# Eight one-column VectorE instructions moved to later tiles, and three lists of waits put in another order, in a two-layer kernel on one core

## The reference

```python
# x: (2, 4096, 192) -> causal 7-tap convolution, one softmaxed set of taps for each of 8 groups of 24 channels
w = softmax(weight)                                  # (8, 7)
out[b, s, c] = sum_k w[c // 24, k] * x_padded[b, s + k, c]
x = out.reshape(8192, 192)
# layer 1
h = x @ w_in                                         # 192 -> 2048
g = h * clip(h + 3, 0, 6) / 6
x = g @ w_out                                        # 2048 -> 192
# layer 2
h = x @ w_in2
P = a[0] + a[1] * h + a[2] * h**2 + a[3] * h**3
Q = 1 + |b[0]| * |h| + |b[1]| * h**2
g = P / (Q + 1e-6)
return g @ w_out2
```

## Time and profile before

| | before |
|---|---|
| median of 3 runs | 1202.07 us |
| profiled execution, its own time | 1204.0 us |
| its span | 1201.9 us |
| PE busy in the span | 1186.5 us, 99% |
| VectorE (DVE) busy | 1160.7 us, 97% |
| ScalarE (ACT) busy | 1065.5 us, 89% |
| GpSimd (POOL) busy | 1072.9 us, 89% |
| granted TensorE clock, mean | 0.998 |

### The profile page before, as it was taken

One profiled execution on the slowest core, in us unless ns is written; L12 is line 12 of the kernel. 1 busy time (PEld: TensorE's weight loads), 2 busy tenths in 40 slices (PEclk: granted clock), 3 DMA queues, 4 the chain that ended last, 5 costly groups with the idle time before them and its releaser, 6 DMA issues. The chain is left out here.

```text
span 1201.9 us, 17842 instructions
## 1 busy us (share of the span) xinstructions
PE 1186.5 (99%) x5145; PEld 963.2 (80%) x5145; DVE 1160.7 (97%) x1784; ACT 1065.5 (89%) x1980; POOL 1072.9 (89%) x829
## 2 busy tenths in 40 slices
PE   8999999999999999999999999999999999999998
PEld 6778888888888888888888888888888888888754
DVE  7999999999999999999999999999999999998898
ACT  7888899898998988989998899889999899888886
POOL 5989989898998989999898998999989899898874
PEclk9999999999999999999999999999999999999999
DMA  4400000000000000010000000000000000000010
GB/s 147 152 2 10 1 23 1 23 10 23 1 1 24 9 23 1 1 32 1 22 1 15 17 2 23 1 23 10 1 23 1 23 1 1 14 1 14 1 44 13
DMA packets 11313, 22.02 MB, mean 18 GB/s; under 512 B 1744, under 2 KB 3152, under 8 KB 11216
## 3 DMA queue, kind: packets, MB, share of 16 engines
q1 hardware_dynamic: 10928, 20.89, 5.9%
q10 hardware_dynamic: 288, 0.01, 0.0%
HBM read 14.60 MB, written 6.29 MB: 17 GB/s over the span
## 5 line engine op out<-in xcount | busy, mean ns | idle before, releaser
L525 POOL TENSOR_TENSOR den<-den,sqr 128x512 f32<-128x512 f32 x246 | 360.7, 1466 | 92.3 <-ACT den L499 91.1
L599 POOL TENSOR_TENSOR g_lo<-g,g_hi 128x512 fp32r<-128x512 f32 x246 | 319.4, 1298 | 7.9 <-ACT g_hi L605 7.9
L492 POOL TENSOR_TENSOR g_lo<-r,g_hi 128x512 fp32r<-128x512 f32 x235 | 309.9, 1319 | 1.7 <-ACT g_hi L605 1.3
L605 ACT ACTIVATE g_hi<-g 128x512 fp32r<-128x512 f32 x246 | 155.9, 634 | 54.9 <-PE y1b_acc L385 47.1
L529 ACT ACTIVATE rsq<-den 128x512 f32<-128x512 f32 x246 | 155.0, 630 | 45.6 <-POOL den L525 42.7
L519 DVE SCALAR_TENSOR_TENSOR num<-h,monic,num 128x512 f32<-128x512 f32 x246 | 184.6, 751 | 8.2
L513 DVE SCALAR_TENSOR_TENSOR num<-h,monic,sqr 128x512 f32<-128x512 f32 x246 | 183.2, 745 | 0.0
L552 DVE SCALAR_TENSOR_TENSOR h<-num,monic,h 128x512 f32<-128x512 f32 x238 | 178.3, 749 | 0.2
L478 DVE SCALAR_TENSOR_TENSOR r<-r,h 128x512 f32<-128x512 f32 x235 | 160.4, 683 | 14.2 <-ACT r L471 13.4
L545 DVE SCALAR_TENSOR_TENSOR den<-den,h 128x512 f32<-128x512 f32 x238 | 161.9, 680 | 1.0 <-ACT h L541 0.9
L574 DVE SCALAR_TENSOR_TENSOR g<-den,h 128x512 f32<-128x512 f32 x238 | 161.1, 677 | 0.2
(11 more groups left out here) (182 smaller groups left out, 2886.8 us busy)
## 6 DMA issues: line engine op xcount, KB each, us to landing
stage_w<-w_pack SPq DMA_DIRECT2D x16, 448.0 KB, 3.4
raw_a<-x_a SPq DMA_DIRECT2D x16, 259.0 KB, 3.2
out<-y_a SPq DMA_DIRECT2D x16, 256.0 KB, 2.0
out<-y_b SPq DMA_DIRECT2D x16, 128.0 KB, 2.3
raw_b<-x_b SPq DMA_DIRECT2D x14, 129.5 KB, 2.7
r<-w_pack SPq DMA_DIRECT2D x4, 96.0 KB, 2.0
raw_b<-x_b SPq DMA_DIRECT2D x4, 65.5 KB, 4.6
y_a<-w_pack SPq DMA_DIRECT2D x2, 96.0 KB, 2.3
```

The source lines that it names most:

```text
L492: eng.tensor_tensor(g1_lo[t % 2][:, :], gated(t)[:, :], f32(g1_hi[t % 2][:, :]), ALU.subtract).then_inc(S["g1lo"], 1)
L525: eng.tensor_tensor(den_of(t), den_of(t), sqr_of(t), ALU.add).then_inc(S["den_sum"], 1)
L599: eng.tensor_tensor(g2_lo[t % 2][:, :], g2[t % 2][:, :], f32(g2_hi[t % 2][:, :]), ALU.subtract).then_inc(S["g2lo"], 1)
L605: return eng.activation(dst, src, ACT.Copy)
```

## The change

The seven entries of the set-up functions leave VectorE's START list, where they stood at the front (side, safe, inverse, c2), behind `gate1` (ratio, c01, scale) and belonged to steps 5, 6, 7, 8, 9, 10 and 11. They are now at the end of VectorE's BEGIN list, in steps 12 to 18. Three functions name their waits in another order.

```diff
-    "vector": [("monic_side", 5), ("monic_safe", 6), ("monic_inverse", 7), ("monic_c2", 8), ("gate1", 0), ("monic_ratio", 9),
-             ("monic_c01", 10), ("monic_scale", 11), ("conv_b1", AHEAD, (2, 2, 2, 3, 5, 6, 7), 1), ("g1lo", 1),
+    "vector": [("gate1", 0), ("conv_b1", AHEAD, (2, 2, 2, 3, 5, 6, 7), 1), ("g1lo", 1),
              ("conv_a", AHEAD, (0, 3, 5, 7, 8, 10))],
...
-             ("x2b_res", SUM1, 0), ("g1lo", 1), ("x2b_lo", SUM1, 0), ("conv_a", AHEAD, (6, 4, 4, 16, 4, 5))],
+             ("x2b_res", SUM1, 0), ("g1lo", 1), ("x2b_lo", SUM1, 0), ("conv_a", AHEAD, (6, 4, 4, 16, 4, 5)),
+             ("monic_side", 12), ("monic_safe", 13), ("monic_inverse", 14), ("monic_c2", 15), ("monic_ratio", 16),
+             ("monic_c01", 17), ("monic_scale", 18)],
...
             if t in full:
+                wait_g(eng, t)
                 eng.wait_ge(d_w_full, 16 * len(full))
-                wait_g(eng, t)
...
         def num2(eng, t):
+            eng.wait_ge(S["abs2"], t + 1)
             eng.wait_ge(S["sq2"], t + 1)
-            eng.wait_ge(S["abs2"], t + 1)
...
         def g_neg(eng, t):
             if (t in on_gpsimd) != (eng is nc.gpsimd):
                 return
-            eng.wait_ge(S["newton"], t + 1)
-            eng.wait_ge(S["g_first"], t + 1)
+            if eng is nc.gpsimd:
+                eng.wait_ge(S["less_two"], gpsimds(t))
             if t - 2 in full:
                 eng.wait_ge(S["n2_done"], t - 1)
             else:
                 after(eng, S["g2lo"], splits(t - 2))
+            eng.wait_ge(S["newton"], t + 1)
+            eng.wait_ge(S["g_first"], t + 1)
             if eng is nc.gpsimd:
-                eng.wait_ge(S["less_two"], gpsimds(t))
                 eng.tensor_tensor(g2[t % 2][:, :], den_of(t), raw_quotient(t), ALU.mult) \
```

## The result

The changed kernel takes 1205.47 us (median of 11 runs, 1204.91 to 1208.37). The kernel before had 1202.14 us in the same measurement. The ratio is 1.0033, with a 95% interval of 1.0024 to 1.0043. The change makes the kernel 3.3 us slower, beyond the bound of 2.4 us named above, and the time lies outside the predicted range.

A forecast was written before the change was run, and what follows sets the result against it. TensorE was taken to bound the stretch from 100 to 600 us and VectorE the last sixteen tiles. The terms -0.1 + 0.7 + 0 = +0.6 us on 1202.07 gave 1202.7 us, with a range of 1201.3 to 1204.2 us.

The forecast's parts named there:

- What bounds the kernel: TensorE from 100 to 600 us, VectorE in the last sixteen tiles; a TensorE delay taken earlier can't be won back.
- Part 1: Set-up leaving steps 5 to 11: a TensorE near miss at 36.67 us goes, gain 0.1 us, bounds 0 and 0.3.
- Free instructions: Steps 12, 13, 14 and 18: monic_side, monic_safe, monic_inverse and monic_scale cost TensorE's wait for x2b_lo nothing.
- monic_c2, 0.1 us: Step 15 on VectorE: fits a bubble in the old phase, taken as 0.1 us, at worst 0.87.
- monic_ratio, 0.4 us with a bound of 0.81: Step 16: takes a wait for GpSimd and conv_b behind it waits again, 0.07 to 0.81 us, taken as 0.4.
- monic_c01, 0.3 us: Step 17, two instructions: fit the bubble in the old phase; 0.3 us with the phase moved, at worst 1.05.
- The 0.1 us of air at `x2b_res`, subtracted: VectorE at 56.16 us: x2b_res starts 0.72 us after the gate, not 0.60, so some 0.1 us absorbs delay.
- Sum of part 2: Set-up entering steps 12 to 18 delays x2b_lo: 0.1 + 0.4 + 0.3 - 0.1 = 0.7 us, bounds about 0 and 2.7.
- TensorE then passes it to the end one for one: A delay of x2b_lo, awaited by TensorE's matmul at 58.35 us, reaches the kernel's end in full.
- Part 3: Order of the waits on GpSimd, VectorE and TensorE: 0 us, with bounds of 0.5 us to both sides.
- The first one: Rival, step 15 to x2b_lo: every two-input instruction meets a long GpSimd one, 2.6 us, 1204.7 us in all; chance 12%.

The follow-up runs named there:

- e8_before_one: The kernel before, set-up in steps 5 to 11 and old order of waits, with the one-input forms of e4_one_input: 1201.62 us, ratio 0.9993.
- e4_one_input: The changed kernel, same places, with the five two-input set-up instructions given one tensor input and a pointer scalar: 1201.78 us, ratio 1.0002 against the kernel before.
- e6_ratio: e4_one_input with monic_ratio back in its two-input form: median 1204.68 us, ratio 1.0020 against the kernel before.
- e7_c01: e4_one_input with the two instructions of monic_c01 back in two-input form: median 1202.96 us, ratio 1.0005 against the kernel before.
- e3_fill: The changed kernel with nine matmuls of no use put in TensorE's wait for x2b_lo: 1203.77 us, ratio 1.0013 against the kernel before.
- e1_waits: Only the changed order of the waits, set-up left in steps 5 to 11: 1202.04 us, ratio 0.9999 against the kernel before.
- e5_late: The changed kernel, two-input forms kept, with monic_ratio and monic_c01 moved to step 18: 1202.49 us, ratio 1.0004 against the kernel before.
- e10_hold: e4_one_input with three reductions of no use on VectorE in step 17, ahead of x2b_lo: 1207.25 us, ratio 1.0040 against the kernel before.
- e12_again: The changed kernel, unaltered, run once more for a second profile: a single execution of 1205.05 us.

## Why the prediction was wrong, point by point

- *What bounds the kernel.* Right. From 100 to 1100 us TensorE is busy throughout in both, and the last 50 us are as full as before: VectorE is busy 39.82 of the 40 us from 1150 us on in both profiles.
- *Part 1, a gain of 0.1 us.* Too small to be told from nothing in the times. The near miss that it rests on is gone: from 33 to 38 us all matmuls of the changed kernel start 0.22 to 0.23 us apart. `e8_before_one`, which shortens L968 and leaves the places, is 0.5 us faster in the median, with an interval that includes no change.
- *Free instructions.* Right for `monic_side` and `monic_inverse`. `monic_safe` took 0.74 us in the changed kernel and still vanished in an idle time. Wrong, by a little, for `monic_scale`: the gate behind it has no time to spare. TensorE's next product waits 0.19 us for it in `e4_one_input` and not at all in `e8_before_one`.
- *monic_c2, 0.1 us.* Right: 0.21 us inside its bubble.
- *monic_ratio, 0.4 us with a bound of 0.81.* This term failed, and its bound too: 1.15 us against the one-input form (`e6_ratio`), 1.20 against the kernel before (3.78 - 2.58). The mechanism was right, that the small instruction takes the wait and hands a second one to `conv_b`. What it left out is that two `conv_b` stand behind it. The delay pushed the second one into GpSimd's long instruction of 50.71.
- *monic_c01, 0.3 us.* Mis-sized: 0.90 us in the changed kernel, inside its bound of 1.05; 0.59 in another phase (`e7_c01`).
- *The 0.1 us of air at `x2b_res`, subtracted.* Not there: the gate and `x2b_res` start 0.72 us apart after the change as before it (55.20 and 55.92). A delay moves both.
- *Sum of part 2, 0.7 us, bound 2.7.* It was 2.05 us against `e4_one_input`, as the start of the waiting matmul shows. In time, with the clock kept up, the changed kernel is 1.7 us slower than the one before (`e3_fill`, 1203.77 against 1202.11), where the forecast had 0.6. So the terms were too small by a factor of nearly three, but this time still lies inside the range, below 1204.2.
- *"TensorE then passes it to the end one for one".* This is the step whose failure moved the time out of the range. It holds for the delay itself, as `e3_fill` shows. But the wait of 2.4 us brought the clock down to half, and that cost 1.7 us in the median on top (1205.47 - 1203.77). The forecast had this cost at nothing, and none of its signs of being wrong looks at the clock. The prediction read the granted clock in its windows, at 1.00 in all of the rows shown, and did not ask what a longer wait would do to it. The profile of before had an example outside those rows: behind waits of TensorE of 1.10 and 0.61 us, which end at 10.15 and 11.96, its clock is at half from 12.5 to 15.9 us. (The changed kernel has 0.82 and 0.61 us there, and the clock at 1.00.)
- *Part 3, nothing.* Right (`e1_waits`).
- *The rivals.* The first one, that the two-input instructions meet long ones of GpSimd, is what happened, with a little less delay than its 2.6 us and the clock's share above it. It was given 12% and should have had more: of the four steps with such instructions three waited (0.74, 0.59 and 1.15 us) and one did not (0.21). The rule of the Trainium skill behind it ("SBUF — State Buffer", section "Who interferes with whom"), the exclusive lock of the shared ports, agrees with the ends of L975 and L615 (55.21 and 55.19 us) and with `e4_one_input`.

## What to carry to other kernels

A one-column VectorE instruction costs 0.1 to 0.2 us, or up to 1.2 us, by whether it has two tensor inputs in SBUF while GpSimd is at work; a pointer scalar in place of the second input took the wait away in the old steps (`e8_before_one`) and in the new ones (`e4_one_input`). When such an instruction is put ahead of others with two inputs, each of them may wait again, so count the followers. And a delay that lets TensorE stand still can cost more than its own length: look at whether a stall of that length anywhere in the trace is followed by a lower granted clock, and put that into the sum.

## What the runs showed that was not expected

TensorE's wait in this place differs from run to run, and its clock with it. With waits of 0.34, 0.38, 0.85 and 1.22 us (`e5_late`, `e4_one_input`, `e7_c01`, `e1_waits`) the profiled execution had 1.00 throughout the stretch. With 1.46, 2.17, 2.35 and 2.36 us (`e6_ratio`, `e10_hold`, `e12_again` and the changed kernel) it fell to 0.50 each time, between 0.6 us before the end of the wait (the changed kernel) and 1.2 us behind it (`e6_ratio`). In the first three of these it was back at about 62 us and in the last at about 64. Nine matmuls without use in the wait, with a rest of 0.31 us, kept it up. They cost nothing and won 1.7 us in the median.

The length of the wait alone does not decide it. Three of the ten runs of `e6_ratio` kept a mean clock of 1.000. A wait of 1.85 us for a gate stands in both profiles: in `e6_ratio` it ends at 77.37 and the clock falls at 78.9, in the changed kernel it ends at 79.12 and the clock stays at 1.00. And in each of these runs TensorE has another wait of 0.6 to 0.8 us (for `y_a`) only three matmuls ahead of the one for `x2b_lo`. What decides is not shown.

The kernel before has runs near 1204 us among those near 1202. Its profiled execution was one, with the clock at half from 12.5 to 15.9 us. The profiled execution of `e1_waits` at 1203.56 us had the clock at 1.00 and instead a wait of 1.22 us for `x2b_lo`, with `conv_b` x2 at 2.88 us beside GpSimd. So there are two ways into such a run; those of the kernel before have a mean clock of 1.000 in some (1204.18) and of 0.998 in others (1203.92). No execution of the kernel before near 1202.1 us was profiled. The eleven runs of `e8_before_one` have none near 1204, but that the one-input forms prevent them is not shown: `e4_one_input` has the same forms and three such runs in ten, each with a mean clock of 0.998 or 0.999.
